# Two-stage mixer kernel: token-major keys with transposed maxima, doubled key and value buffers, and other places for the first token load and the weight units

## The reference

```
q_s = exp(q - max_d q);  q_s /= sum_d q_s + 1e-9          # softmax over the 64 of a head
k_s = exp(k - max_s k);  k_s /= sum_s k_s + 1e-9          # softmax over the 576 tokens
attn = q_s @ (k_s^T @ v)                                  # per head
x  = attn as [8, 576, 512]
u  = x + (relu(x^T @ w_tok1) @ w_tok2)^T                  # mixing over tokens, 256 hidden
y  = u + relu(u @ w_ch1) @ w_ch2                          # channels, 1536 hidden (stage B)
out = y + relu(LN(y) * g @ w2_ch1) @ w2_ch2               # channels, 2048 hidden (stage C)
```

## Time and profile before

| | us |
|---|---|
| median of 3 runs (1586.39 to 1592.27) | 1591.9 |
| the profiled execution's own time | 1593.26 |
| its span, first to last instruction | 1591.5 |
| PE busy | 1488.4 (94%) |
| DVE busy | 1091.0 (69%) |
| ACT busy | 698.0 (44%) |
| POOL busy | 308.3 (19%) |
| moved by DMA | 429.28 MB, mean 270 GB/s |

### The profile page before, as it was taken

How to read it: one execution, slowest core, us unless ns; L and a number is a source line. 1 busy time by engine, 2 the same in 40 slices (tenths; PEclk the granted TensorE clock), 3 DMA queues, 4 the chain that set the end, 5 groups by cost and what they waited for, 6 DMA issues and landing times.

```text
span 1591.5 us, 19837 instructions
## 1 busy us (share of the span) xinstructions
PE 1488.4 (94%) x7584; PEld 1332.6 (84%) x7584; DVE 1091.0 (69%) x1165; ACT 698.0 (44%) x844; POOL 308.3 (19%) x315
## 2 busy tenths in 40 slices
PE   6999977889989989999989999999999999999998
PEld 5998876778878867878978888888888888889998
DVE  7988866497379378388588578568757865873276
ACT  5656644353353354254353454245335434532342
POOL 5687775431213122220000000000000000000000
PEclk9999988999999999999999999999999999999999
DMA  8889885998879988988757767876876687667766
GB/s 242 255 296 288 285 286 188 391 332 324 314 281 339 341 309 301 344 326 304 264 206 269 248 233 240 266 253 204 281 239 244 225 268 247 222 218 244 258 211 202
DMA packets 150334, 429.28 MB, mean 270 GB/s; under 512 B 14240, under 2 KB 43488, under 8 KB 150240
## 3 DMA queue, kind: packets, MB, share of 16 engines
q1 hardware_dynamic: 132768, 361.94, 66.5%
q0 software_dynamic: 17472, 66.07, 11.6%
HBM read 348.26 MB, written 79.69 MB: 269 GB/s over the span
## 4 chain that ended last, share of the span: by engine, by line
PE 70%; DVE 12%; DMA 10%; issue 4%; ACT 2%; POOL 1%; SPq 1%; DVEq 0%; ACTq 0%; POOLq 0%
PE ps L1132 23%; PE ps L1134 22%; PE ps L1133 22%; DMA w_ring<-w_scratch_B 7%; DVE x_lo L833 2%; DVE o_lo L981 2%; DMA qt<-q 2%; DVE q_sum L760 1%; POOL q_lo L461 1%; PE ps L1156 1%; PE ps L1167 1%; DVE h L967 1%; DVE qt L777 1%; DVE h L951 1%; DVE q_den L768 1%
## 5 line engine op out<-in xcount | busy, mean ns | idle before, releaser
L1132 PE MATMUL ps<-o_hi,w_ring 128*128 128x462 f32 (+1 forms) x980 | 371.0, 379 | 34.9 <-DVE o_lo L981 22.9
L1132 PE MATMUL ps<-x_hi,w_ring 128*128 128x462 f32 (+1 forms) x980 | 368.7, 376 | 22.4 <-DMA w_ring<-w_scratch_B 11.7
L1133 PE MATMUL ps<-o_lo,w_ring 128*128 128x462 f32 (+1 forms) x980 | 367.4, 375 | 0.0
L1134 PE MATMUL ps<-x_hi,w_ring 128*128 128x462 f32 (+1 forms) x980 | 367.3, 375 | 0.0
L1134 PE MATMUL ps<-o_hi,w_ring 128*128 128x462 f32 (+1 forms) x980 | 367.0, 375 | 0.0
L1133 PE MATMUL ps<-x_lo,w_ring 128*128 128x462 f32 (+1 forms) x980 | 366.8, 374 | 0.0
L674 ACT CAST o_hi<-h 128x924 fp32r<-128x924 f32 (+1 forms) x210 | 202.0, 963 | 264.5 <-PE ps L1134 225.5
L981 DVE TENSOR_TENSOR o_lo<-h,o_hi 128x924 fp32r<-128x924 f32 (+1 forms) x210 | 247.0, 1179 | 65.3 <-ACT o_hi L674 65.2
L1132 PEld LDWEIGHTS ps<-o_hi,w_ring 128*128 128x128 f32 x980 | 186.7, 191 | 70.1 <-issue 33.5
L1132 PEld LDWEIGHTS ps<-x_hi,w_ring 128*128 128x128 f32 x980 | 186.2, 190 | 51.4 <-issue 23.2
L951 DVE TENSOR_TENSOR h<-ps,h 128x924 f32<-128x924 f32 (+1 forms) x90 | 100.5, 1117 | 174.5 <-PE ps L1134 174.2
(11 more groups left out here) (140 smaller groups left out, 1842.7 us busy)
## 6 DMA issues: line engine op xcount, KB each, us to landing
w_ring<-w_scratch_C SPq DMA_DIRECT2D x280, 512.0 KB, 3.8
w_ring<-w_scratch_B SPq DMA_DIRECT2D x210, 512.0 KB, 5.5
w_scratch_C<-w_out POOLq DMA_DIRECT2D x8, 1792.0 KB, 10.9
w_scratch_C<-last_pair POOLq DMA_DIRECT2D x8, 1792.0 KB, 11.6
w_scratch_B<-w_out POOLq DMA_DIRECT2D x6, 1792.0 KB, 9.4
w_scratch_B<-last_pair POOLq DMA_DIRECT2D x6, 1792.0 KB, 9.7
kt<-kT SPq DMA_DIRECT2D x32, 288.0 KB, 6.2
u_scratch<-u_out SPq DMA_DIRECT2D x32, 288.0 KB, 4.9
```

What stands on the lines that cost most here:

```text
L1132: mm(dst, a_hi, b_hi, start=start, stop=False, skip_group_check=onto)
L1133: mm(dst, a_hi, b_lo, start=False, stop=False, skip_group_check=onto)
L1134: return mm(dst, a_lo, b_hi, start=False, stop=stop, skip_group_check=onto)
```

## The change

kT is gone, from the arguments, the buffers and SP's queue. k and v have two buffers each, by the batch's parity, and are loaded two batches ahead. The key maximum is now taken from the token-major k tile: one DVE reduction over four token tiles, whose reads are 2 KB apart in a partition, then a maximum with the fifth (half) tile, four PE transposes into bank 0, one DVE reduction of 512 numbers, and the four spreading transposes as before. At step 4 SP loads chunks 0 and 1 of the first tokens; chunks 2 and 3 come after the first four weight entries, once the last maximum and the last `r` product are done. `tok_raw`, `k_part` and `kv` live in xn, where those chunks go. `sum_x(0,0)` waits for two chunks. `hi_unit(7)` stands behind ACT's last step, `hi_x(0, 4..6)` each behind one of the first three takes. `HI_AT` is new. What is left out below: declarations, memsets and indices for the second buffers.

```diff
-    HI_AT = {1 + 5 * i: UNITS_A + i for i in range(U0["C"] - UNITS_A)}
-    HI_AT.update({22 + 9 * i: U0["C"] + i for i in range(UNITS["C"])})
+    HI_AT = {e: UNITS_A + i for i, e in enumerate((0, 4, 8, 12, 27, 36))}
+    HI_AT.update({(s + 1) * ENTRIES["B"] + e: UNITS_A + 6 + 5 * s + i
+                  for s in range(3) for i, e in enumerate((0, 6, 11, 27, 36))})
...
 # SP
+            def load_k(b):
+                wait(sp, kv_done, b - 1)
+                for t, rows in ST:
+                    sp.dma_start(ke[0:rows, b % 2, t, :], k[b, t * P:t * P + rows, :]).then_inc(k_in[b % 2][t], 16)
...
             def step(i, later):
-                    for t in range(3):
-                        if not first:
-                            load_k(i + 1, ST[t:t + 1])
-                        load_q(i + 1, ST[t:t + 1])
...
-                    load_v(i + 1)
-                    load_kT(i + 2)
+                if later >= 1:
+                    load_q(i + 1, ST[0:2])
+                if later >= 2:
+                    load_k(i + 2)
+                if later >= 1:
+                    load_q(i + 1, ST[2:])
+                if later >= 2:
+                    load_v(i + 2)
...
-            load_kT(0)
-            load_k(0, ST)
+            load_k(0)
             load_v(0)
-            load_kT(1)
...
+            load_k(1)
+            load_v(1)
             for i in range(NB - 1):
+                if i == NB // 2:
+                    sp.wait_ge(u_stored, 16 * NC * 2)
+                    for c in range(2):
+                        load_x(0, c)
                 step(i, 2 if i < NB - 2 else 1)
...
-            sp.wait_ge(u_stored, 16 * NC * 2)
-            for c in range(NC):
-                load_x(0, c)
             for n in range(RW):
                 load_entry(n)
+            sp.wait_ge(x_in, 32)
+            sp.wait_ge(kcol_done, NB)
+            sp.wait_ge(r_done, ND * NB)
+            for c in range(2, NC):
+                load_x(0, c)
             step(NB - 1, 0)
 # ACT
             def step(i, later):
-                    if later:
-                        exp_k(i + 1, ST[0:1])
...
-                    exp_k(i + 1, ST[1:2])
+                    exp_k(i + 1, ST[0:1])
...
-                    exp_k(i + 1, ST[2:3])
+                    exp_k(i + 1, ST[1:3])
...
                     if later == 0 and c == 1:
-                        hi_unit(i)
                         hi_x(0, 3)
...
-            for p in (4, 5, 6):
-                hi_x(0, p)
+            hi_unit(NB - 1)
             for c in CALLS:
                         if p in (0, 1, 2, 6):
                             take(c, p)
+                        if c.index == 0 and p < 3:
+                            hi_x(0, 4 + p)
 # DVE
+            def max_k(b):
+                for t, _ in ST:
+                    dve.wait_ge(k_in[b % 2][t], 16 * (b // 2 + 1))
+                wait(dve, kcol_done, b)
+                nc.vector.tensor_reduce(k_part[:, :], ke[:, b % 2, 0:NT - 1, :].rearrange("p t c -> p c t"),
+                                        AX.X, ALU.max).then_inc(kpart_made, 1)
+                rows = ST[-1][1]
+                dve.wait_ge(kpart_made, 2 * b + 1)
+                nc.vector.tensor_tensor(k_part[0:rows, :], k_part[0:rows, :], ke[0:rows, b % 2, NT - 1, :], ALU.max)\
+                  .then_inc(kpart_made, 1)
+
+            def max_kcol(b):
+                dve.wait_ge(kcol_done, b + 1)
+                wait(dve, kmax_spread, b)
+                nc.vector.tensor_reduce(k_max[:, :], bank[0][:, :].rearrange("p (c t) -> p c t", c=NC), AX.X, ALU.max)\
+                  .then_inc(kmax_made, 1)
...
             def step(i, later):
                 if first:
-                    max_k(0, range(NC))
+                    max_kcol(0)
...
-                    max_k(1, range(NC))
+                    max_k(1)
                     norm_kv(0)
+                    max_kcol(1)
...
                     lo_qT(i, ST[0:2])
                     if later:
-                        max_k(i + 1, range(2, NC))
+                        max_kcol(i + 1)
...
-                        sub_k(i + 1, ST[0:1])
...
-                        sub_k(i + 1, ST[1:3])
+                        sub_k(i + 1, ST[0:3])
...
                 if later == 2:
-                    max_k(i + 2, range(2))
+                    max_k(i + 2)
...
+            max_k(0)
             reciprocal_q(0, 1)
             norm_q(0, 1)
             batches(step)
 # PE
+            def turn_kmax(b):
+                pe.wait_ge(kpart_made, 2 * (b + 1))
+                wait(pe, ksub_made, NT * b)
+                for c in range(NC):
+                    x = nc.tensor.transpose(bank[0][:, c * P:(c + 1) * P], k_part[:, c * P:(c + 1) * P], ident[:, :])
+                x.then_inc(kcol_done, 1)
...
                 else:
+                    if later:
+                        turn_kmax(i + 1)
                     for c in range(NC):
                         product_g(i, c)
                         transpose_q(i, ST[c + 2:c + 3])
-                        if c == 1 and later:
+                        if c == 2 and later:
                             spread_kmax(i + 1)
```

More of the change, by code:

```diff
@@ L6, with mixer_kernel @@
 Call = namedtuple("Call", "index stage sg pos j n chunks epp e0 g0")
-def mixer_kernel(nc, q, k, kT, v, w_tok1, w_tok2, w1b, w2b, g_ln, w1c, w2c, out):
+def mixer_kernel(nc, q, k, v, w_tok1, w_tok2, w1b, w2b, g_ln, w1c, w2c, out):
     fp32, f32r = mybir.dt.float32, mybir.dt.float32r
@@ L194, in mixer_kernel @@
         tok1_lo_made, tok2_lo_made = sem("tok1_lo_made"), sem("tok2_lo_made")
-        kT_in = [sem(f"kT_in{c}") for c in range(NC)]
-        k_in = [sem(f"k_in{t}") for t in range(NT)]
+        k_in = [[sem(f"k_in{n}{t}") for t in range(NT)] for n in range(2)]
         q_in = [sem(f"q_in{t}") for t in range(NT)]
-        v_in = sem("v_in")
+        v_in = [sem(f"v_in{n}") for n in range(2)]
+        kpart_made, kcol_done = sem("kpart_made"), sem("kcol_done")
         kmax_made, kmax_spread = sem("kmax_made"), sem("kmax_spread")
@@ L273, in _ @@
         def _(sp):
-            def load_kT(b):
-                wait(sp, kmax_made, b * NC)
-                for c in range(NC):
[L277 to L282, removed]
+            def load_k(b):
+                wait(sp, kv_done, b - 1)
+                for t, rows in ST:
+                    sp.dma_start(ke[0:rows, b % 2, t, :], k[b, t * P:t * P + rows, :]).then_inc(k_in[b % 2][t], 16)
             def load_v(b):
-                wait(sp, kv_done, b)
+                wait(sp, kv_done, b - 1)
                 for t, rows in ST:
-                    sp.dma_start(vt[0:rows, t, :, 0:P], v[b, t * P:t * P + rows, :].rearrange("p (c e) -> p c e", c=NC))\
-                      .then_inc(v_in, 16)
+                    sp.dma_start(vt[0:rows, b % 2, t, :, 0:P],
+                                 v[b, t * P:t * P + rows, :].rearrange("p (c e) -> p c e", c=NC))\
+                      .then_inc(v_in[b % 2], 16)
             def load_q(b, chunks, first=False):
@@ L317, in step, with load_x @@
                     sp.dma_start(u_v[:, c, bass.ds(i * S, S)], u_out[:, c, :]).then_inc(u_stored, 16)
+            def load_x(pos, c):
+                if c == 0 and pos >= NSG:
+                    sp.wait_ge(y_stored, 64 * (pos - NSG + 1))
+                if c == 0 and pos > 0:
+                    sp.wait_ge(x_lo_made, 7 * pos)
+                n = 2 * SIZES[pos % NSG]
+                sp.dma_start(xn[:, c * n:(c + 1) * n], tokens(source["BC"[pos // NSG]], pos % NSG)[:, c, :])\
+                  .then_inc(x_in, 16)
             load_q(0, ST, first=True)
@@ L522, in exp_k @@
                     act.wait_ge(ksub_made, b * NT + t + 1)
-                    nc.scalar.activation(ke[0:rows, t, :], ke[0:rows, t, :], ACT.Exp).then_inc(kexp_made, 1)
+                    nc.scalar.activation(ke[0:rows, b % 2, t, :], ke[0:rows, b % 2, t, :], ACT.Exp).then_inc(kexp_made, 1)
             def exp_q(b, chunks):
@@ L556, in hi_x @@
                 if p == 0:
-                    act.wait_ge(x_in, 64 * (pos + 1))
+                    act.wait_ge(x_in, 64 * (pos + 1) if pos > 0 else 32)
                     if pos >= NSG:
@@ L589, in step @@
                     hi_qT(i, ST[3:4])
-                    if later:
-                        exp_k(i + 1, ST[0:1])
-                    else:
+                    if later == 0:
                         hi_x(0, 0)
@@ L734, in _ @@
         def _(dve):
-            def max_k(b, chunks):
-                for c in chunks:
-                    dve.wait_ge(kT_in[c], 16 * (b + 1))
-                    wait(dve, kmax_spread, b)
-                    nc.vector.tensor_reduce(k_max[:, c:c + 1], kt[:, c, :], AX.X, ALU.max).then_inc(kmax_made, 1)
+            def max_k(b):
[13 more added lines that the diff above has]
+                  .then_inc(kmax_made, 1)
             def sub_k(b, chunks):
                 for t, rows in chunks:
-                    dve.wait_ge(k_in[t], 16 * (b + 1))
```

(8 more changed lines are left out.)

47 lines of the change are left out of this document (16 added, 31 removed).

## The result

The changed kernel takes 1608.3 us (median of 5 runs, 1601.58 to 1610.39) against 1591.9 before. The ratio is 1.0103, with a 95% interval of 1.0076 to 1.0131: slower by 1.0%, where I forecast 1564 us and gave "slower" 0.05.

A forecast was written before the change was run, and what follows sets the result against it. It took stage A to be bound by a loop from q tile through DVE, POOL and unit store to the next q tile. Terms -8.5, 0, -10, -12, +2, -2.3, +3 sum to -27.8: about 1564 us, range 1549 to 1584.

The forecast's parts named there:

- the paragraph on the maxima: Stage A: DVE's new key maxima take 3.0 us a step for 1.39, mostly covered; +2 us, between 0 and +8.
- the loop over q: Stage A: q tile, DVE, POOL's split, subtractions and unit store, then the next q tile; 28.7 us a step.
- rival 4: Strided reads in `max_k` are slow: twice the price gives 1576 us, chance 0.06; four times 1609, far end's chance 0.05.
- Step 0: Start of stage A: `max_k(0)` ahead of `norm_q` costs 3.0 us uncovered; +3 us, between +1 and +4.
- The seam's -8.5: End of stage A: early x chunks save PE's 7.97 us wait and 2.7 of slow clock, less 2.1.
- The seam's count of POOL's chain: ACT's copies moved: POOL is serial, entry 3 follows at X+29, X being the start of `hi_unit(6)`; 0 us, -9 to +4.
- Halves that meet: Positions 1 to 3: moved units remove two thirds of PE's waits and slow clock; -12 us, between -19 and 0.
- The -10 of units 8 to 11: Entries 0 to 24: earlier copies remove SP's 9.2 us wait on unit 11's store; -10 us, between -13 and 0.
- rival 2: The seam is DMA-bound: units outpace the engines, the 10 us become waits for the ring; 1574 us, chance 0.18.
- the loads' -2.3: Stage A: 1.15 MB a batch fewer, v and k a batch ahead, waits for them go; -2.3 us, between -9 and 0.

The follow-up runs named there:

- e1: The changed kernel with the maxima's four PE transposes behind PE's first product of the step, and DVE's reduction of their result one place later: 1609.5 us, ratio 1.0116.
- e2: The changed kernel with DVE's key maxima moved from the end of a step to behind its `r_lo` subtractions: 1594.8 us, ratio 1.0026.
- e3: The changed kernel with the reduction of 2048 numbers reading neighbours instead of numbers 2 KB apart, without the true key maximum: 1598.3 us in one run.
- e5: The kernel before with the new table of units and all four chunks of the first tokens loaded at step 4: 1573.7 us, ratio 0.9873.
- e4: The kernel before with only the new table of entries for the weight units: 1578.4 us, ratio 0.9915.
- e10: As e6, but the first position's units at their old entries 1, 6, 11, 16, with 12 and 13 at 27 and 36: 1575.2 us, ratio 0.9900.
- e6: As e5, with the change's order of ACT's copies at the seam: 1574.6 us, ratio 0.9889 to the kernel before.

## Why the prediction was wrong

**The step that failed** is the paragraph on the maxima, which put +2 us, "most is covered by the loop", where the six steps grew by 32.3. Three things in it were wrong, in the order of their weight.

First, what the new wait holds. I wrote that the four transposes "fall into a wait" and costed their 0.45 us. But they are a wait, on DVE's maxima, at the head of PE's queue; and by my own count DVE was through at 164.87 + 3.0 = 167.9, when PE stood at them at 166. I gave that to the loop over q, in which I had put DVE only up to `norm_q`. e1 shows that the place on PE is not the cause: behind the first product the same time is waited for `lo_qT`. e2 gets 13.5 us back by the place on DVE, a lower price of the half tile's maximum included. DVE works without a pause from the q tile's landing to `lo_qT`. Work put at the end of that row holds PE back, PE's products and transposes then hold back the next `r`, and `r` starts DVE's row anew. In this round, 20.9 us on DVE and 13.1 on PE, the last q tile and the store ahead of it hardly occur (2.7 us of DVE's waits), so the store could cover nothing.

Second, the reduction's price: 3.75 us, not 2.3. It was rival 4's mechanism, and I gave it 0.06 + 0.05 on the ground that no row spoke against neighbours' prices. At twice the price I let 1.5 us of 2.2 show; the runs show 1.66 times, and it is in each of eight maxima, 8 x 1.49 = 12 us of DVE's time. What of this shows in the whole no run gives by itself, since in e3 the half tile's maximum fell too. By rival 4's own rate (1.5 us shown of 2.2) the reduction would have cost 8 us in all, so its price alone does not make the loss.

Third, the half tile's maximum: 2.61 us, not 0.7. The earlier trace rows had a `sum_x` of 2.32 us with POOL beside it, and I used that for `sum_x` alone. The earlier trace rows have POOL's store at 172.92, directly behind its subtractions, which the timeline of the kernel before has here:

```profile
168.42 4.20 POOL L431 TENSOR_TENSOR last_pair<-w_op,last_pair 128x1024 fp32r<-128x1024 f32 x2
```

That is half a microsecond behind the 167.9 at which my maxima ended, so any delay of them meets it. POOL's `lo_q` stands there even without a delay: in e3, with the reduction at the price that I had put, the half tile's maximum still took 1.66 us beside it. I did not put the two together.

The two prices together made 6.3 us of 3.0, and behind the wait of 5.2 us PE's clock was at its lower level, which cost 2.7 us a step and was not in the count at all.

**Step 0** was +6.8 for +3. The trace has the same work there: 4.4 us ahead of `norm_q` (3.70 + 0.68), then 4.9 of batch 1 ahead of `norm_kv`. e3, with the cheaper reduction, gets 2.2 us of it back; the rest is not taken apart.

**The other terms.** The seam's -8.5 was -11.7; e5, which adds the early load to e4, has -8.6 in this stretch against e4, so the term was right for what it counted and the other 3 us are not explained. The seam's count of POOL's chain held to 1 us (entry 3 at X + 28.7 for X + 29). Halves that meet gave -16.1 for -12; their waits went nearly all, while in e4 the whole stretch gained only 7.9. The -10 of units 8 to 11 were -2.6, and the 18 entries behind them took 4.2 us more: rival 2 was right there. e10 shows it by itself: the longest wait for a store on SP's queue was worth under 2 us. That PE loses the rest to full DMA queues either way is the reading that fits; no run moved the bytes out of this stretch. Of the loads' -2.3 the waits of PE for v are gone from the trace, but no run isolates them.

With the key path and the loads of k and v as they were, the new table, ACT's new order and an early load of the first tokens (e6), the kernel is 1.1% faster than before. What the changed kernel has beyond that costs 1608.3 - 1574.6, some 34 us, and takes all of it back. It is the key path, but with it the two buffers for k and v, the new order of loads, and the late load of chunks 2 and 3, where e6 loads all four early; no run has these without the new key path.

## What to carry to other kernels

Before putting work on an engine, find the stretch in which it runs without idle time into something that gates the loop: there a microsecond costs a microsecond or more, and when the added work is long enough, another loop than the one you found becomes the longest. A wait added at the head of a queue is priced by what stands behind it, not by the instruction that waits. A transfer that closes a loop should not be issued behind a large one of another queue: moving one store by a step was worth as much as any part of this change.

## What the runs showed of the hardware

- A DVE reduction of 2048 fp32 numbers to 512 took 3.75 us reading at 2 KB steps (3.70 to 3.91 over two kernels) and 2.26 us reading neighbours.
- A DVE maximum of two SBUF tiles of 64x512 took 0.68 us alone and 2.61 us with a POOL subtraction beside it; the reduction with one input took 3.70 us alone and 3.76 us beside POOL.
- With a 1792 KB store and a unit's loads of POOL's queue under way, POOL's queue had 85.6% of the DMA engines' time and SP's 15.6%. The packets were nearly equal in number, 545 against 466, but carried 2.10 against 0.37 MB; a 128 KB q tile landed in 7.2 us there, and in 3.9 to 4.6 us with the store elsewhere.
- Towards the end of a PE wait of 5.2 us the granted clock fell from 1.00 to 0.50, its 1.2 GHz level, and was back at 1.00 after 5.3 us of work; over the step of 34 us the mean is 0.90.
